# Splitting the second weights of the second expert layer: all remainders and half of the casts on GpSimd, the other half of the casts on ScalarE

## The reference

```python
expert_idx = np.argmax(logits, axis=1)
gate_w = probs[np.arange(N), expert_idx]
for e in range(E):
    mask = expert_idx == e
    h = np.maximum(x[mask] @ w1[e], 0.0)
    out[mask] = gate_w[mask, None] * (h @ w2[e])
```

## Time and profile before

| | us |
|---|---|
| median of 3 runs | 1659.91 |
| lowest and highest | 1656.42 to 1662.17 |
| the profiled execution, its own time | 1657.15 |
| span of its trace | 1655.4 |
| PE busy | 1569.5 |
| DVE busy | 611.0 |
| ACT busy | 470.0 |
| POOL busy | 324.8 |

### The profile page before, as it was taken

The page is one execution under the profiler, slowest core; times in us unless marked ns, Lnnn a source line. Parts: engine busy times, 40 slices in busy tenths (PEclk is TensorE's granted clock), DMA queues, the critical chain, the costliest instruction groups (busy, mean ns, idle before and its releaser), DMA issues.

```text
span 1655.4 us, 21247 instructions
## 1 busy us (share of the span) xinstructions
PE 1569.5 (95%) x7516; PEld 1309.9 (79%) x7517; DVE 611.0 (37%) x1021; ACT 470.0 (28%) x864; POOL 324.8 (20%) x527
## 2 busy tenths in 40 slices
PE   5999999999999999999999999999999992799997
PEld 5999998788888888888888888888888771677775
DVE  4788788342211211211211311311122244554224
ACT  3777777112111111111111211211111132554123
POOL 3445444200300300210020030030030004422102
PEclk7999999999999999999999999999999995899999
DMA  5565555100110110110110110020020014654310
GB/s 133 149 158 146 140 146 175 56 1 0 59 44 1 52 49 0 51 51 0 51 51 0 51 51 0 4 98 0 0 100 3 0 52 163 248 181 156 121 40 24
DMA packets 50405, 115.94 MB, mean 70 GB/s; under 512 B 7862, under 2 KB 9910, under 8 KB 50368
## 3 DMA queue, kind: packets, MB, share of 16 engines
q1 hardware_dynamic: 44480, 102.49, 19.6%
q10 hardware_dynamic: 3488, 6.66, 1.4%
q0 software_dynamic: 2400, 6.31, 1.0%
HBM read 81.58 MB, written 13.40 MB: 57 GB/s over the span
## 4 chain that ended last, share of the span: by engine, by line
PE 85%; DVE 4%; issue 3%; DMA 3%; POOL 3%; ACT 1%; SPq 1%; POOLq 0%; DVEq 0%; ACTq 0%
PE psum L391 24%; PE psum L393 24%; PE psum L392 24%; PE psum L624 3%; PE psum L613 2%; PE psum L637 2%; PE psum L638 2%; PE psum L614 1%; DMA w_raw<-in_moe_w_dram 1%; PE psum L595 1%; DVE row_min L1116 1%; PE psum L649 1%; DMA out_dram<-y_row,idx_now 1%; PE psum L829 1%; POOL x_sorted L530 1%
## 5 line engine op out<-in xcount | busy, mean ns | idle before, releaser
L974 ACT ACTIVATE h_hi<-psum 128x512 fp32r<-128x512 f32 x192 | 115.1, 599 | 867.4 <-PE psum L393 867.4
L391 PE MATMUL psum<-xt_lo,w_hi 128*128 128x512 f32 x768 | 304.0, 396 | 0.2 <-DVE xt_lo L1207 0.2
L393 PE MATMUL psum<-xt_hi,w_lo 128*128 128x512 f32 x768 | 301.1, 392 | 0.0
L391 PE MATMUL psum<-w_lo,h_hi 128*128 128x512 f32 x768 | 300.0, 391 | 0.0
L393 PE MATMUL psum<-w_hi,h_lo 128*128 128x512 f32 x768 | 299.3, 390 | 0.0
L392 PE MATMUL psum<-w_hi,h_hi 128*128 128x512 f32 x768 | 298.8, 389 | 0.0
L392 PE MATMUL psum<-xt_hi,w_hi 128*128 128x512 f32 x768 | 298.7, 389 | 0.0
L1292 DVE SCALAR_TENSOR_TENSOR h_lo<-psum,h_hi 128x512 fp32r<-128x512 f32 x192 | 132.8, 692 | 360.8 <-ACT h_hi L974 360.7
L424 POOL CAST w_hi<-w_raw 128x512 fp32r<-128x512 f32 x64 | 40.0, 625 | 813.3 <-PE psum L393 804.1
L1335 DVE SCALAR_TENSOR_TENSOR tok<-psum,route,tok 128x512 f32<-128x512 f32 x84 | 57.5, 745 | 384.6 <-PE psum L393 384.6
L393 PEld LDWEIGHTS psum<-xt_hi,w_lo 128*128 128x128 f32 x768 | 144.2, 188 | 33.6
(11 more groups left out here) (236 smaller groups left out, 1906.4 us busy)
## 6 DMA issues: line engine op xcount, KB each, us to landing
w_raw<-in_moe_w_dram SPq DMA_DIRECT2D x32, 2048.0 KB, 8.1
k_hh<-k_hi SPq DMA_DIRECT2D x32, 192.0 KB, 3.0
x_sorted<-zeros SPq DMA_DIRECT2D x21, 257.0 KB, 3.7
x_row<-x_sorted ACTq DMA_DIRECT2D x19, 256.0 KB, 2.8
k_raw<-in_k_dram SPq DMA_DIRECT2D x8, 384.0 KB, 3.0
v_raw<-in_v_dram SPq DMA_DIRECT2D x16, 192.0 KB, 3.4
k_b<-k_lo SPq DMA_DIRECT2D x16, 192.0 KB, 3.3
q_raw<-in_q_dram SPq DMA_DIRECT2D x7, 384.0 KB, 3.8
```

The source lines that it names most:

```text
L391: pe.matmul(acc, a[0], b[1], start=start, stop=False)
L393: return pe.matmul(acc, a[1], b[0], start=False, stop=stop)
L974: act.activation(h_s[0][:, f, :], psum[:, f % 4, :], ACT.Relu).then_inc(m1.h_hi, 1)
```

## The change

ACT casts only the first four pieces of w2 of each expert of the second layer. POOL makes all eight remainders, and casts the last four pieces itself, each right before its remainder. DVE's `w2_lo2` is gone. Three places that waited for both engines (SP twice, PE once) now wait for POOL's count of eight. Apart from that, `turn_h(i, 1)` stands one step earlier in PE's down product, after f = 0 instead of after f = 1.

```diff
@@ sync
-        sp.wait_ge(m2.w2_lo, HF)
-        sp.wait_ge(s_w2_pool, KF - HF)
+        sp.wait_ge(s_w2_pool, KF)
         sp.wait_ge(s_xrow, 16)
         sp.dma_start(w2_raw[:], m2.wb[1]).then_inc(m2.w2_in, 16)
...
-            sp.wait_ge(m2.w2_lo, HF * e)
-            sp.wait_ge(s_w2_pool, (KF - HF) * e)
+            sp.wait_ge(s_w2_pool, KF * e)
             sp.dma_start(w2_raw[:], m2.wb[e]).then_inc(m2.w2_in, 16)
@@ gpsimd
         def w2_lo2(e, u):
-            for f in range(HF, KF):
-                pool.wait_ge(m2.w2_hi, KF * e + f + 1)
+            for f in range(KF):
+                if f < HF:
+                    pool.wait_ge(m2.w2_hi, HF * e + f + 1)
+                else:
+                    copy(w2_p[u][0][:, f, :], w2_raw[:, f, :]).then_inc(s_w2_pool_hi, 1)
+                    pool.wait_ge(s_w2_pool_hi, (KF - HF) * e + f - HF + 1)
                 pool.tensor_tensor(w2_p[u][1][:, f, :], w2_raw[:, f, :], w2_p[u][0][:, f, :].bitcast(F32),
                                    ALU.subtract).then_inc(s_w2_pool, 1)
@@ tensor
-                pe.wait_ge(m2.w2_lo, HF * (e + 1))
-                pe.wait_ge(s_w2_pool, (KF - HF) * (e + 1))
+                pe.wait_ge(s_w2_pool, KF * (e + 1))
...
-                    if f == 2:
+                    if f == 1:
                         turn_h(i, 1)
@@ scalar
         def w2_hi2(e, u):
             act.wait_ge(m2.w2_in, 16 * e + 16)
-            for f in range(KF):
+            for f in range(HF):
                 act.copy(w2_p[u][0][:, f, :], w2_raw[:, f, :]).then_inc(m2.w2_hi, 1)
@@ vector
-        def w2_lo2(e, u):
-            for f in range(HF):
-                dve.wait_ge(m2.w2_hi, KF * e + f + 1)
-                dve.tensor_tensor(w2_p[u][1][:, f, :], w2_raw[:, f, :], w2_p[u][0][:, f, :].bitcast(F32),
-                                  ALU.subtract).then_inc(m2.w2_lo, 1)
...
-        w2_lo2(0, 0)
...
-        w2_lo2(1, 1)
...
-                w2_lo2(e + 2, u)
```

More of the change, by code:

```diff
@@ L258, in program @@
     m1, m2 = Phase("m1", w1, w2), Phase("m2", m2w1, m2w2)
+    s_w2_pool, s_w2_pool_hi = sem("m2_w2_split_pool"), sem("m2_w2_hi_pool")
     HF = KF // 2
-    s_w2_pool = sem("m2_w2_split_pool")
     s_chain = sem("route_step")
```

## The result

| | before | after |
|---|---|---|
| median, us | 1661.04 (4 runs, 1656.42 to 1663.55) | 1697.61 (4 runs, 1695.98 to 1699.57) |
| ratio to before, 95% interval | | 1.0232 (1.0210 to 1.0254) |
| the profiled execution, us | 1657.15 | 1699.57 |
| span of its trace, us | 1655.4 | 1697.9 |
| mean granted clock | 0.977 | 0.965 |

The change is slower by 36.6 us in the medians, and by 42.4 us between the two profiled executions, which is the pair that the terms of the prediction are compared with. The profiled execution of before lay 3.9 us under its median, that of after 2.0 over it.

The account below looks back on a forecast made before the run. Until tile 4 a ring of load, ACT casts and POOL's split bounds the second expert layer, then PE. Terms 40.1, 7.45, 0.5, 0.45, 2.1 and 1.7 sum to 52.3 us; 1657.15 becomes 1709.5, called 1710, range 1690 to 1722.

Parts of the forecast that it names:

- the one without a clash: Rival: in the new overlap DVE and POOL do not hold each other up (0 for 3.5 us): 1695.5 us; chance 0.17.
- the clash: POOL's split beside DVE's w1 remainders of the next expert: the two take turns, adding 3.5 us to POOL (0 to 4.63).
- down product of tile 4 starts later by: Second expert layer up to tile 4: longer rings and the store behind POOL's split move this start from 1480.2 to 1520.3, 40.1 us.
- tiles 7 to 9: Two tiles after an expert's end: 30.6 us against 30.13, +0.5; DVE no longer delays g_row, but tile 9 awaits its store.
- tiles 14 to 16: Two tiles after an expert's end, with POOL's split and a store of 8.6 us: 30.6 us against 28.51, +2.1.
- The two regimes: Second expert layer: experts 0 to 3 wait for weights; from tile 4 on PE is the bound, apart from gaps at expert ends.
- the ring: Early experts: w2 load, ACT's casts, POOL's split, next load, as there is one raw tile; from 17.6 to 26.9 us.
- POOL's split: POOL's four subtractions plus four pairs of cast and subtraction for each expert's w2: 13.0 us, 12.7 for the first, without clash.
- Load to cast: From the start of a w2 load to ACT's first cast of it: 8.9 us for the first, 9.7 in each ring.
- the still longer ring that was a rival: Rival: next w1 load queued right behind w2's, or slowing stores, adds one us per load: 1718 us and up; chance 0.1.
- The store, 8.6 us each: POOL's store of a tile, queued behind its split; ACT's y_row waits 8.6 us from the store's first instruction.
- The clock: PE behind each new pause: the lower clock costs 1.7 us, taken from the 2.85 us pause in tile 8.

Follow-up runs that it names:

- e7: Kernel before with the transposes of h's second half after f = 0, and DVE making all eight w2 remainders of every expert, POOL none: 1660.45 us, ratio 1.0011.
- e8: Kernel before with earlier transposes, DVE making all eight w2 remainders for experts 0 to 3 alone, shared with POOL for 4 to 7: 1645.03 us, ratio 0.9933.
- e3: Changed kernel, but SP holds back the w2 loads of experts 5, 6 and 7 until ACT made y_row of tiles 4, 6 and 9: 1684.69 us, ratio 1.0167.
- e11: Changed kernel with all eight w2 casts back on ACT and the late w2 loads of experts 5 to 7: 1652.62 us, ratio 0.9975.
- e4: Kernel before with only the transposes of the second half of h moved up to after f = 0: 1646.18 us, ratio 0.9935.
- e12: Second run of the kernel before with nothing but the earlier transposes: 1647.85 us, ratio 0.9945.
- e6: Kernel before with earlier transposes, DVE's four remainders kept, the four upper w2 casts moved from ACT to POOL: 1671.43 us, ratio 1.0084.
- e5: Changed kernel, but ACT makes all eight w2 casts again and POOL keeps all eight remainders: 1662.42 us, ratio 1.0028.
- e2: Changed kernel, but DVE starts an expert's w1 remainders only when POOL has made all w2 remainders of the expert before: 1684.34 us, ratio 1.0162.
- e10: Kernel before, transposes as they were, but POOL starts its four w2 remainders only when DVE has made its four: 1652.47 us, ratio 0.9983.

## Why the prediction was right, and where its sizes were off

The direction, the mechanism and the range held. The loss was forecast nearly a quarter too large, 52.3 us against 42.4 between the profiled executions, and the median of 1697.6 lies below the 1700 to 1712 that I had called likeliest. By the time alone the nearest case would have been the one without a clash (1695.5), and that would be the wrong reading: the clash is there, 3.85 us a ring, and other terms were too large. The terms, from the starts of the down products in the two profiled executions:

| term | before | forecast | measured |
|---|---|---|---|
| down product of tile 4 starts later by | | 40.1 | 35.1 |
| tiles 4 to 7 | 38.9 | 46.35 | 46.15 |
| tiles 7 to 9 | 30.1 | 30.6 | 31.6 |
| tiles 9 to 14 | 63.9 | 64.4 | 65.2 |
| tiles 14 to 16 | 28.5 | 30.6 | 26.1 |
| behind the pause of tile 16 | | 1.7 | -0.2 |
| sum of the loss | | 52.3 | 42.5 |

- *Bound now.* The two regimes and the ring were read rightly as long as the ring grows. That it is set by POOL's share alone was too much: e7 and e8 show two other limits right below it.
- *POOL's split.* 12.72 us against 13.0 forecast. The clash, 3.85 against 3.5, and DVE's four pieces 7.26 against "7 us or more". The prediction gave the undisturbed `g_lo` by a row (1548.27) at which POOL was not splitting; the changed kernel has it inside a split, at 1495.30 and 1499.27, 0.69 us each, so the reading holds. In the 7.26 us of DVE's four pieces POOL did 3.41 us of its own work (7.26 - 3.85), with DVE's 4.63 together 8.04: so some 0.8 us did run side by side. By the Trainium skill (SBUF — State Buffer, Who interferes with whom), in which the engine that comes second is blocked fully, the clash would be all of DVE's 4.63 us, an estimate; the trace agrees with that rule but for about a sixth. The very first split lost only 1.9 us of 3.5 to the clash, as most of it was over when DVE's remainders began.
- *Load to cast.* I took 8.9 and 9.7 us; 8.44, 8.73, 9.82 and 8.71 were measured. In the last three cases the next w1 load left 0.9 us behind that of w2, and the still longer ring that was a rival for this reason didn't come. With the first split this makes the casts of expert 4 start at 1492.04 instead of 1495.9, 3.9 of the 5.0 us by which the term at tile 4 was too large.
- *The store, 8.6 us each: the step that was sized wrong.* From the copy to `y_row` 7.6 (tile 4), 7.7 (tile 6) and 9.0 us (tile 9), and 3.6 at tile 16, from 1678.67 to 1682.27. The two stores that I took the 8.6 from both lay beside a weight load (e3), and behind tile 15 there is none left to load. These 5.0 us are the whole miss at tiles 14 to 16 (4.5), and e3 showed the same at tiles 4, 6 and 9. At tile 4 the store was 1.0 us shorter than forecast, most of what else was missing there. From tile 7 to 9 the term was 1.0 us too small: the store was 0.4 longer than forecast, and the split took 13.4 us, as DVE's last w1 remainders reached into its start. As the pause before tile 16 then became short, its 1.7 us of low clock fell away too.
- *The clock.* PE's timeline behind the pause at tile 9, a plain matmul before, at and after the point where its clock returns:

```profile
1597.85 0.63 PE L389 MATMUL psum<-w_odd_lo,g_hi 128*128 128x512 f32 x1
...
1598.28 0.58 PE L390 MATMUL psum<-w_odd_hi,g_hi 128*128 128x512 f32 x1
1598.70 0.40 PE L391 MATMUL psum<-w_odd_hi,g_lo 128*128 128x512 f32 x1
1598.93 0.40 PE L389 MATMUL psum<-w_odd_lo,g_hi 128*128 128x512 f32 x1
```

  Matmuls start 0.43 us apart up to 1598.28 and 0.23 apart from 1598.70 on. The granted clock is 0.50 from 1593.02 to 1598.70, the lower level (1.2 GHz), and 1.00 behind it. I had taken 1.7 us behind each pause, from that of 2.85 us. Against the same tiles of e11, which have no pause of over 0.6 us ahead of them, tile 9 took 15.1 us instead of 12.5 (behind a pause of 6.42 us), tile 4 14.6 instead of 12.5 (4.75 us) and tile 6 13.8 instead of 12.3 (5.13 us): 2.6, 2.1 and 1.5 us. From tile 4 to tile 6 the forecast 32.3 us was met by luck: more of the lower clock (0.4 us) and longer hand-overs made up for the store (0.9) and the split (0.3), which were shorter.
- *The earlier transposes.* 12.52 us a tile against 12.54 forecast, and no wait for `g_row` at tiles 8 and 15. What I had not seen is that the same edit alone would be worth 11 us in the kernel before (e4, e12). In the change this gain is hidden behind the stores.
- *What the change gives back.* DVE's and ACT's lighter loads gave nothing that can be seen, as forecast: PE waited for POOL.

Put together: four kernels have the earlier transposes and differ only in the two halves of the change to the split.

| | casts on ACT | four casts on POOL |
|---|---|---|
| DVE keeps four remainders | e4, 1646.2 | e6, 1671.4 |
| POOL makes all remainders | e5, 1662.4 | after, 1697.6 |

The remainders alone cost 15 to 16 us, the casts alone 25, and both together 49 to 51, 9 to 10 more than the sum of the two. The turns (e2) and the slow stores (e3) are 11 to 13 us each; they are what the longer split runs into, so they lie inside these 50 us and must not be added to them.

## What to carry to other kernels

An operation moved to an idle engine is costed by what waits for that engine last. Here POOL was busy for 20% of the span, but each microsecond of its split was paid in every ring and once more ahead of the next store. When an engine's queue also holds stores that free a buffer, look what else is on the DMA queues while they run. And test the parts of a change alone: its small second edit was a gain of 0.6%, hidden by the loss of the first, and the two halves of the first cost more together than one by one.

## What the hardware showed that I had not expected

- An indirect store of 128 rows of 2 KB took 3.5 to 3.9 us from the copy of its row numbers until the buffer was free, and 7.6 to 9.0 us when a 2 MB load had left 0.2 to 0.6 us ahead of it.
- Two loads of 2 MB, the second 4.7 us behind the first: the second took 13.1 us instead of 9.7 (e7). A load of 2 MB that left 0.9 us behind the other did not delay the first one, which took 8.7 to 9.8 us (the changed kernel).
- DVE's subtractions with two inputs in SBUF and POOL's operations slow each other on both sides: 4.63 to 7.26 us on DVE, 12.72 to 16.57 on POOL, casts too. When their starts are some tenths of a us apart, it depends on these who is held up: POOL's first subtraction (2.17 us, with DVE's piece at 0.68) or DVE's pieces (1.80 and 1.75, with POOL's at 1.35), in e4 and in the kernel before. Making either engine wait for the other was faster each time that it was tried (e2: 12 to 13 us, e10: 3 to 5 us).
